# Transposes of a hidden activation, each done as two halves of 64 tokens in the two row halves of TensorE

## What is computed

```python
# 1. attention, 4 batches x 8 heads x 576 tokens x 64: a pooled one (factor 4) plus a local one (|i-j| < 4)
x = (out_up + out_local)  -> 2304 tokens x 512
# 2. gated feed-forward, 512 -> 1536 -> 512
gate = 1.0 / (1.0 + np.exp(-(x @ w_gate)))
val = x @ w_val
h = gate * val
x = h @ w_out
# 3. soft mixture of 8 experts with 4 slots each, over all tokens
logits = x @ phi                      # 2304 x 32
d = softmax over tokens, c = softmax over slots
slot_input = d.T @ x                  # 32 x 512
slot_out = relu(slot_input @ w1) @ w2 # per expert
out = c @ slot_out
```

## Time and profile before

| | us |
|---|---|
| median of three runs | 594.77 |
| lowest and highest | 593.92, 596.26 |
| the profiled execution, its own time | 594.65 |
| its span in the trace | 592.9 |
| TensorE busy in it | 549.3 (93%) |
| weight loads of TensorE busy | 412.9 (70%) |
| VectorE, ScalarE, GpSimd busy | 224.3, 200.1, 101.5 |

### The profile page before, as it was taken

One profiled execution on the slowest core, in us unless ns is written; L12 is line 12 of the kernel. 1 busy time (PEld: TensorE's weight loads), 2 busy tenths in 40 slices (PEclk: granted clock), 3 DMA queues, 4 the chain that ended last, 5 costly groups with the idle time before them and its releaser, 6 DMA issues.

```text
span 592.9 us, 11279 instructions
## 1 busy us (share of the span) xinstructions
PE 549.3 (93%) x4486; PEld 412.9 (70%) x4486; DVE 224.3 (38%) x500; ACT 200.1 (34%) x514; POOL 101.5 (17%) x171
## 2 busy tenths in 40 slices
PE   6787998999999999999999999999999999968963
PEld 5666777777778778777877878787787777824432
DVE  3696851444625252444235244542212220130103
ACT  4554754334243233152324234233233111230103
POOL 7855022141231202121121202110000000000000
PEclk9697999999999999999999999999999999999988
DMA  8567942121220211111020200102504167589958
GB/s 193 151 139 197 340 119 59 43 72 32 64 71 11 61 23 41 43 42 43 21 63 1 63 20 22 23 21 59 228 1 148 66 237 257 202 310 393 400 190 318
DMA packets 86707, 70.97 MB, mean 120 GB/s; under 512 B 61312, under 2 KB 65920, under 8 KB 86656
## 3 DMA queue, kind: packets, MB, share of 16 engines
q1 hardware_dynamic: 86656, 70.25, 37.8%
HBM read 65.52 MB, written 4.72 MB: 118 GB/s over the span
## 4 chain that ended last, share of the span: by engine, by line
PE 83%; DMA 5%; DVE 4%; issue 2%; ACT 2%; POOL 1%; SPq 1%; POOLq 0%; ACTq 0%; DVEq 0%
PE gateb L940 26%; PE valb L940 25%; PE unitb L948 4%; PE unitb L897 3%; DMA ew_low<-in_moe_w_dram 3%; PE unitb L853 3%; PE unitb L860 2%; PE unitb L962 2%; PE unitb L979 2%; PE unitb L888 2%; PE unitb L868 2%; PE unitb L1023 2%; PE unitb L875 2%; PE unitb L881 1%; PE gateb L1041 1%
## 5 line engine op out<-in xcount | busy, mean ns | idle before, releaser
L940 PE MATMUL gateb<-w_hl,xhl 128*128 128x512 f32 x648 | 163.5, 401 | 0.6 <-ACT xhl L588 0.6
L940 PE MATMUL valb<-w_hl,xhl 128*128 128x512 f32 x648 | 162.2, 399 | 0.0
L940 PEld LDWEIGHTS gateb<-w_hl,xhl 128*128 128x128 f32 x648 | 119.3, 190 | 33.6 <-issue 8.9
L940 PEld LDWEIGHTS valb<-w_hl,xhl 128*128 128x128 f32 x648 | 118.6, 188 | 23.8 <-issue 0.2
L659 ACT ACTIVATE hid<-gateb 128x512 f32<-128x512 f32 x54 | 32.3, 598 | 170.1 <-PE gateb L940 170.1
L779 DVE SCALAR_TENSOR_TENSOR hid<-hid,valb 128x512 f32<-128x512 f32 x54 | 37.1, 688 | 126.6 <-PE valb L940 126.6
L577 POOL TENSOR_TENSOR vd<-v 72x256 f32<-72x256 f32 x16 | 12.1, 756 | 168.8 <-PE unitb L881 166.5
L588 ACT ACTIVATE hT<-unitb 128x512 f32<-128x512 f32 x54 | 32.0, 597 | 21.2 <-PE unitb L948 21.2
L948 PE MATMUL unitb<-ident,hid 128*128 128x128 f32 x216 | 33.3, 278 | 2.5 <-DVE hid L779 1.7
L762 DVE TENSOR_TENSOR xraw<-unitb,outd 128x192 f32<-128x192 f32 x43 | 15.0, 356 | 53.3 <-PE unitb L897 53.1
L948 PEld LDWEIGHTS unitb<-ident,hid 128*128 128x128 f32 x216 | 24.3, 140 | 7.7 <-issue 4.1
(11 more groups left out here) (174 smaller groups left out, 665.7 us busy)
## 6 DMA issues: line engine op xcount, KB each, us to landing
ew_low<-in_moe_w_dram SPq DMA_DIRECT2D x19, 1024.0 KB, 13.6
ew_high<-in_moe_w_dram SPq DMA_DIRECT2D x13, 1024.0 KB, 7.8
qtok<-in_q_dram SPq DMA_DIRECT2D x32, 144.0 KB, 2.8
ktok<-in_k_dram SPq DMA_DIRECT2D x32, 144.0 KB, 3.0
v<-in_v_dram SPq DMA_DIRECT2D x32, 144.0 KB
out_dram<-outs SPq DMA_DIRECT2D x18, 256.0 KB, 3.0
vloc<-in_v_dram SPq DMA_DIRECT2D x32, 112.0 KB
xraw<-in_moe_w_out_dram SPq DMA_DIRECT2D x12, 256.0 KB, 5.8
```

The lines of the kernel that those rows point to most:

```text
L940: last = mm(bank[:, :], xhl[:, i % NX, x, kk, :], w_hl[:, c, m, w, kk, :], start=j == 0, stop=j == len(order) - 1)
```

## The change

Each TR step becomes two, `TR0` for the tokens 0 to 63 of a tile and `TR1` for 64 to 127, and each has a bank of its own. TensorE issues both when it comes to TR0: eight transposes of 64 rows x 128 columns of `hid` against a 64 x 64 identity, alternately in the upper and the lower half of the array's rows, and it waits for both banks before the first. ScalarE copies the halves one after the other, 128 x 256 each. Each later use of the ring of four banks is moved on, since 54 more steps take a place in it. Nothing else in the list of steps changes.

```diff
 UNITS = (... "PV1", "PV2",
-         "WT", "GP", "GS", "TR", "LG", "LS", "ELT", "SL")
+         "WT", "GP", "GS", "TR0", "TR1", "LG", "LS", "ELT", "SL")
+
+SECOND = {"TR0": "TR1"}
...
+    def tr(i, c):
+        return ("TR0", (i, c)), ("TR1", (i, c))
     for i in range(t0):
         for c in range(chunks):
-            put(place_of[("val", (i, c))] + 1, ("TR", (i, c)))
+            put(place_of[("val", (i, c))] + 1, *tr(i, c))
...
# ScalarE
-            elif name == "TR":
+            elif name in ("TR0", "TR1"):
                 i, c = arg
                 wait_unit(act, s)
...
-                copy(hT[:, 4 * c:4 * c + 4, t * P:(t + 1) * P], ub[:, :].rearrange("p (f n) -> p f n", f=4)).then_inc(free, 1)
+                tok = slice(t * P + HEADS[part].start, t * P + HEADS[part].stop)
+                copy(hT[:, 4 * c:4 * c + 4, tok], ub[:, 0:4 * QT].rearrange("p (f n) -> p f n", f=4)).then_inc(free, 1)
...
# TensorE
+            if name in SECOND:
+                other = (SECOND[name], arg)
+                wait_free(pe, reuse=other)
+                both = (ub, banks[at[other][1]])
...
-            elif name == "TR":
+            elif name == "TR0":
                 i, c = arg
                 pe.wait_ge(hid_done, ff_n[arg] + 1)
                 for j in range(4):
                     f = 4 * c + j
-                    last = nc.tensor.transpose(ub[:, j * P:(j + 1) * P], hid[:, i % NH, f * P:(f + 1) * P], ident[:])
-                last.then_inc(unit_ready, 1)
+                    last = [nc.tensor.transpose(b[:, j * QT:(j + 1) * QT], hid[rows, i % NH, f * P:(f + 1) * P], ident[rows, rows])
+                            for b, rows in zip(both, HEADS)]
+                for done in last:
+                    done.then_inc(unit_ready, 1)
```

## The result

The changed kernel takes **609.10 us** (median of four executions, 607.62 to 610.81) beside 595.14 for the kernel before: ratio 1.023, 95% interval 1.0204 to 1.0256. That is 14.0 us slower, where 9.4 was forecast. It lies in the stated range of 598 to 614, but above the 600 to 608 that the prediction gave for its own mechanism; the room up to 614 had been left for rival 2. A second measurement gave 608.89 beside 595.54, ratio 1.0236 (1.0183 to 1.0290).

What follows compares the result with a forecast made beforehand. TensorE was taken to bound the kernel from 62 to 520 us. Shape changes 4.7, nothing behind tiled steps, bank waits 3.1 and tile 16 1.9, less 0.3, gave +9.4 on 594.65: about 604.0 us, range 598 to 614.

Steps and rivals of the forecast that it cites:

- rival 2: At the transposes: the halves queue up or each load takes 0.11; +10.6 to 12.7 us, 615 to 617; chance 0.14.
- What bounds the kernel: TensorE from 62 to 520 us: what it saves or adds is the kernel's time, one for one.
- Rival 3: At TensorE's wait for weights (16.95 us): it takes the delay, so no change, 594.7 us; chance 0.06.
- The price of the halves: At each TR (transposing step): 0.06 us a pair of halves, 0.24 a step, 0.20 less than four times 0.11.
- The price of the shape: Two shape changes cost 0.37 us: +0.15 at each of 31 TR steps between full-array steps, 4.7; nothing behind tiled steps.
- Rival 1: At the halves: a change of rows alone costs nothing; result -3.5 us, 591.1; chance 0.10.
- The bank waits: Waits for the second bank: eight places, together 3.5 us, counted as +3.1; tile 16 another +1.9.
- 0.3 each: At TR (2, 0), S1 and PdT1 of head pair 10: 0.3 us each left of waits of 0.9 to 1.2.
- at the full clock of 1.00: TensorE from 142 to 410 us: busy 265.77 of 268 us at the 2.4 GHz level in the profile before.
- The range: Whole kernel: 600 to 608 us for the forecast itself; 598 to 614 stated, to leave out no more than 0.2.
- ScalarE: The copies of the halves: 8.6 us more work, costed at nothing, as ScalarE is idle 66% of the span.

Runs made afterwards that it cites:

- experiment 1: The changed kernel again, no edit, for another profile: 608.89 us, ratio 1.0236.
- experiment 5: The changed kernel with row halves in 41 of the 54 transposing steps; the other 13 keep full transposes in one bank: 598.64 us, ratio 1.0078.
- experiment 4: The changed kernel with both halves taken from the upper row half of the array; banks, copies and counts the same: 620.62 us, ratio 1.0425.
- experiment 2: The changed kernel with full 128x128 transposes, two into each of two banks, and no row halves: 603.79 us, ratio 1.0138.
- experiment 9: The kernel before again, no edit, for another profile: 595.13 us, ratio 0.9993.
- experiment 3: The changed kernel with the four transposes of the upper row half first, then the four of the lower: 607.23 us, ratio 1.0191.

## Why the prediction was right, and where it was not

**What bounds the kernel: right.** Each delay ahead of the last `val` arrived at the end: 16.2 and 16.1 us in the changed kernel, 15.6 and 15.0 in experiment 1, 9.6 and 9.5 with only the banks, 3.9 and 3.9 in experiment 5. Rival 3 is out.

**The price of the halves: right.** A pair takes 0.06; side by side it saves 0.25 us a step against the same rows (experiment 4). Rival 2 is out.

**The price of the shape: right**, and its open point, whether a change of rows alone costs as much, is closed: +0.14 a step between full-array steps, nothing behind a tiled one. The saving of 0.20 meets two changes of 0.35 together, where the prediction had 0.37: the streaming alone would have given -0.20, and with full transposes in the same two banks (experiment 2) a lone step grows by 0.00. The Trainium skill ("TensorEngine Tiling (Array Packing)", Key Properties) lets every changed mode drain the engine; for rows alone the trace now agrees, with these numbers. Rival 1 is out.

**The bank waits: right in place, low in size.** All nine places waited. The growth is 6.7 us where 5.4 was worked out (experiment 2). The term that was lowest is the "0.3 each" of the three places where the next step had waited already: 0.41, 0.65 and 0.41 came, 0.6 us of the 1.3. The other six each came 0.06 to 0.2 above their term. The prediction took off 0.1 at four of these places, because the emptying of the array hides in a wait. That was right in kind: where the clock held, the eight places grow in the changed kernel by as much as with full transposes, to 0.03 us, so the change of shape cost next to nothing there.

**The step that failed** is "at the full clock of 1.00": I read the clock off the profile of before and costed each wait at its own length. The changed kernel puts idle times of 1.4 to 1.7 us at TR (2, 0), TR (2, 2) and tile 16, and behind the last two the clock was at 0.50 for 3.4 us in part of the executions, 1.5 to 1.6 us more each. The profile of before has two idle times of this kind (1.49 and 1.45 us ahead of L881) whose clock had held, so its rows gave no price; the profile of experiment 9 gives it. The fixed part is 10.5 where 9.4 was forecast, and some 3.5 us of the median's 14.0 are left. The waits at TR (2, 2) and tile 16 would give 3.1 us of it if the clock fell behind both in every execution, and it did not. That the rest is the clock is inferred, since a profile shows the falls of one execution and not those of the median, and it may not be all: the execution of experiment 1 with the highest mean clock, 0.981, still took 607.11 us.

**The range.** The sum and the direction held, and their parts were confirmed one by one, but 609.10 lies outside the 600 to 608 of the forecast itself; it is inside the stated range only because that one was widened towards rival 2, which did not happen. That it fell inside is in part luck. The prediction's own terms (31 changes at 0.12 to 0.18, the waits at half to one and a quarter of 5.0) give 600.6 to 606.2 and not up to 608.

**ScalarE: right to cost it at nothing by itself.** It is busy 204.2 of 609.0 us; its copies count only in the bank waits above.

## What to carry to other kernels

A small tile shape in TensorE pays only if its steps stand beside steps of the same or another small shape: a visit from full-array work costs two changes, 0.35 us together here, and this is more than the 0.20 us that the halves save of a 0.45 us step. Counting the changes in the list of steps, and putting full-array steps together, took off 5.7 us (1%) without touching a single matmul, 4.2 us of it by the changes and 1.1 by two waits that went. A resource from a ring (here a bank) that one step takes twice moves the reuse of all later ones, and a new wait on a full TensorE is priced with what the clock did behind waits of its length elsewhere in the traces.

## What the runs showed of the hardware that I had not expected

TensorE reorders across row halves: of eight transposes written upper four first, the lower ones begin mostly within 17 ns of the upper ones, and the fourth of the list begins as the seventh or eighth in all 54 steps. The clock fell behind a part of the idle times of one and the same length: two of five of 2.15 us, 9 of 28 of 1.45 to 1.65 at the two places that all 14 profiles have, three of five of 1.44 to 1.68 at tile 16 (the changed kernel's two profiles and experiments 2, 3 and 4), and one of twelve of 1.43 at TR (2, 0) and TR (2, 2); behind none of five of 0.88 to 0.94, nor of the 28 of 0.87 ahead of L948. And 64 bytes more per partition ahead of the tiles, never read or written, raised the stream of the experts' weights from 394 to 409 GB/s and made the kernel 0.46% faster (0.29% to 0.63%); what in the addresses does it stays open.
